# Queries and keys of the first units in smaller transfers, and a new order of small steps in the attention ramp

## The chip, the cores and the metric

The kernel runs on one core of a Trainium2 chip. The metric is the device time of one execution in microseconds. The kernel before took 631.29 us, the median of 3 runs (631.18 to 631.58). The profiled execution took 631.73 us.

## The reference

All is float32. Attention over 576 positions, for 2 batches and 8 heads of width 64, sees a window of the last 64 positions. Its output, 1152 tokens by 512, goes through a two-layer network with a softplus, and then through four gated experts with a relu.

```
scores = where(0 <= i - j < 64, q @ k.T / 8, -1e9)
attn   = exp(scores - max);  attn /= sum(attn) + 1e-9
x      = attn @ v                                  # 1152 x 512
h = x @ w_in                                       # 512 -> 2048
y = (max(h, 0) + log1p(exp(-|h|))) @ w_out         # 2048 -> 512
p = probs / (sum(probs) + 1e-9)
out = sum over e of p[:, e] * (max(y @ w1[e], 0) @ w2[e])   # 512 -> 1024 -> 512, 4 experts
```

## The kernel before, in words

**Precision.** A matrix product of the two networks is made of three: each operand is split into a high part (rounded to the format fp32r) and a low part (the rest), and high x high, high x low and low x high are summed. So each operand costs a copy (the high part) and a subtraction (the low part) before TensorE can use it: `split_up` and `up_high` make them for the first layer's weights (`wa`), `split_down` for the second's (`wb`), `x_high` and `x_low` for the attention's output, `hidden_high` and `hidden_low` for the hidden slices.

**Attention.** The work is cut into 24 units, each 192 query positions of one batch and two heads, in three windows of 64 (`w` = 0, 1, 2). Two units are a group of inputs: a row of it holds the queries and keys of the first unit, those of the second, and then the values of both (per partition 2560, 2560 and 3072 bytes; for 128 partitions 320, 320 and 384 KB). A unit goes through the engines so: TensorE `scores` (three products, each two passes) into a PSUM bank; VectorE `masked_scores` adds the mask and reduces to the negated maxima, window by window; ScalarE `softmax_exp`, three exponentials with row sums; GpSimd `add_eps` adds epsilon to the sums (units 2 to 8; VectorE does it for others); VectorE `row_inverse` and, up to unit 10, `normalise_first`; TensorE `transpose_probs`; ScalarE `copy_pT` out of PSUM; TensorE `weigh_values`; ScalarE `x_high`, VectorE `x_low`.

**Order.** Each engine has its own queue, written out by hand, and runs it strictly in order; semaphores join them. TensorE's list (L1137 to L1178) is: scores of units 0 to 2, transposes of 0, and then scores of unit j + 1, weighing of j - 2, transposes of j - 1, and so on. From unit 8 on, pieces of the first layer's matmuls (`start_up`) stand between. Then 48 steps follow, each a hidden slice of the first layer (`up`, 12 matmuls), the scores, transposes and weighing of a later unit while there are any, and the second layer's product of the slice three steps back (`down_width`). The experts follow, 8 times `product` (L1097) and `down_tokens` (L1121).

**Transfers.** SP issues all of them from one queue (L348 to L386). In it stand: unit 0's queries and keys, unit 1's, group 1's queries and keys, group 0's values, group 2 whole, group 1's values, group 3, the first block of `w_in` (two slices of `wa`), group 4, the second block, the first of `w_out`, and group 5, which waits for the weighing of unit 1. The third block of `w_in` takes the buffer of the first, and so waits for both low parts of its two slices.

**The other hands of the ramp.** VectorE copies the high parts of weight slices 0 to 4 behind the normalisation of units 4, 5, 7, 8 and 9 (`FIRST_SPLIT`), and GpSimd makes their low parts in halves (`up_low_half`, L433, called from L452 to L465); in the same loop stands `add_eps(unit + 1)`, behind the half. ScalarE and VectorE split slices 5, 6 and 7 in steps 1, 3 and 4 (`LATE_SPLIT`). In the first three steps (`LAG`) ScalarE makes the previous hidden slice's high part between the exponential and the logarithm of its own step, and VectorE its low part ahead of `relu_ln`.

Of the kernel before, what the change touches and what calls it, by code (L numbers as in the profile page):

```python
# [10 lines left out]
P = 128  # L11
# [10 lines left out]
FT = FB // P  # L22
# [9 lines left out]
N_WARM = 8  # L32
SLOTS = 3
EARLY = 2
SPLIT_GROUPS = 2
Q_COLS = 2 * 3 * P
K_COLS = 2 * (UNIT + WIN)
UNIT_QK = 3 * P + UNIT + WIN
SLOT = Q_COLS + K_COLS + 6 * P
LAG = 3  # L40
# [14 lines left out]
def two_stage_mlp_after_window_attention(nc, units, w_in, w_out, probs, w1, w2, out):  # L55
    ctx = ExitStack()
    with ctx:
# [3 lines left out]
        def sem(name):  # L61
            return ctx.enter_context(nc.semaphore(name))
# [147 lines left out]
        def score_bank(u):  # L210
            return ps_score[u % 2 if u < ALT_SCORED else 0]

        def pT_bank(u):
            return ps[3] if u < ALT_UNITS and u % 2 else ps_pT

# [24 lines left out]
        raw_a_in = [sem(f"raw_a_in{j}") for j in range(2)]  # L240
        raw_b_in = [sem(f"raw_b_in{j}") for j in range(2)]
        unit_landed = [sem(f"unit_landed{i}") for i in range(SLOTS + EARLY)]
        scores_landed = [sem(f"scores_landed{g}") for g in range(SPLIT_GROUPS)]
        first_unit_landed = sem("first_unit_landed")
        gate_in = sem("gate_in")
        out_sent = sem("out_sent")
        warm_zero = sem("warm_zero")
        consts = sem("consts")
        score_done = sem("score_done")
        negmax_done = sem("negmax_done")  # L250
        first_maxima = sem("first_maxima")
        exp_done = sem("exp_done")
        eps_done = sem("eps_done")
# [39 lines left out]

        FIRST_SPLIT = {4: 0, 5: 1, 7: 2, 8: 3, 9: 4}
        EPS_AHEAD = range(2, SCORED - 1)
        LATE_SPLIT = {1: 5, 3: 6, 4: 7}

        def f32(ap):
            return ap.bitcast(F32)
# [11 lines left out]
        def _(sp):  # L311

            def attention_inputs(g):
                s = slot_of(g)
                if g >= SLOTS + EARLY:
                    sp.wait_ge(pv_done, 2 * before_in_slot(g) + 2)
                sp.dma_start(slots[s], units[g]).then_inc(unit_landed[s], 16)

            QK = Q_COLS + K_COLS

            def first_queries_keys(g):
                sp.dma_start(slots[g][:, 0:QK], units[g][:, 0:QK]).then_inc(scores_landed[g], 16)

            def first_values(g):
                sp.dma_start(slots[g][:, QK:SLOT], units[g][:, QK:SLOT]).then_inc(unit_landed[g], 16)
# [19 lines left out]
            def down_in(b):  # L345
                return lambda j: w_out[4 * b + j]

            sp.dma_start(slots[0][:, 0:UNIT_QK], units[0][:, 0:UNIT_QK]).then_inc(first_unit_landed, 16)  # L348
            sp.dma_start(slots[0][:, UNIT_QK:2 * UNIT_QK], units[0][:, UNIT_QK:2 * UNIT_QK]).then_inc(scores_landed[0], 16)
            first_queries_keys(1)  # L350
            first_values(0)
            attention_inputs(2)
            first_values(1)
            attention_inputs(3)
            up_weights(0, up_in(0), (0,))
            attention_inputs(4)
# [41 lines left out]
        def _(pool):  # L398
# [51 lines left out]
            for u in (2, 3, 4):  # L450
                add_eps(u)
            for i, unit in enumerate((4, 5, 6, 7)):  # L452
                if unit in FIRST_SPLIT:
                    pool.wait_ge(wa_hi, FIRST_SPLIT[unit] + 1)
                else:
                    pool.wait_ge(norm_done, unit + 1)
                up_low_half(i // 2, i % 2)
                add_eps(unit + 1)
            for i, unit in zip(range(len(FIRST_SPLIT) - 1, 2 * len(FIRST_SPLIT) - 2), (8, 9, 9, 9)):
                pool.wait_ge(norm_done, unit + 1)  # L460
                if i == 4:
# [17 lines left out]
        def _(act):  # L479
# [116 lines left out]
            for k in range(STEPS):  # L596
                n, f = k // FT, k % FT
                if k < LAG:
                    copy_pT(k + WEIGHED)
                absolute(n, f)  # L600
                if LAG <= k < N_UNITS - WEIGHED:
                    copy_pT(k + WEIGHED)
                exponential(n, f)
                if k > 0:
                    hidden_high((k - 1) // FT, (k - 1) % FT)
                logarithm(n, f)
                if k < LAG:
                    x_high(k + WEIGHED)
                if k < N_UNITS - SCORED:
                    softmax_exp(k + SCORED)  # L610
                if LAG <= k < N_UNITS - WEIGHED:
                    x_high(k + WEIGHED)
                if k in LATE_SPLIT:
                    act.wait_ge(wa_hi, LATE_SPLIT[k])
                    split_up(0, LATE_SPLIT[k])
                if 0 < k - LAG + 1 < FT:
                    split_down(0, k - LAG + 1)
                if n == NCH - 1:
                    split_up(1, f)
                if 0 <= k - (NCH - 1) * FT - LAG - 1 < FT:  # L620
                    split_down(1, k - (NCH - 1) * FT - LAG - 1)
                if k in B_STEPS:
                    b_high(B_STEPS[k])
                if n == NB1 * NCH - 1:
                    a_high(f // 4, f % 4)
# [36 lines left out]
        def _(dve):  # L662
# [9 lines left out]

            def masked_scores(u):

                dve.wait_ge(score_done, u + 1)
                if u >= 3:
                    dve.wait_ge(pT_done, u - 2)
                c, half, _ = unit_place(u)
                first = (2 * c + half) % 3 == 0
                for w in range(3):  # L680
                    m = 0 if first and w == 0 else 1
                    e = dve.tensor_tensor_reduce(prob[:, u % 3, w, :], score_bank(u)[:, P * w:P * w + P],
                                                 mask[:, m, :], -SCALE, BIG, ALU.add, ALU.min,
                                                 negmax[:, u % 3, w:w + 1])
                    if u == 0 and w < 2:
                        e.then_inc(first_maxima, 1)
                e.then_inc(negmax_done, 1)
# [201 lines left out]
            for k in range(STEPS):  # L889
# [2 lines left out]
                    masked_scores(k + SCORED)  # L892
                if k < LAG:
                    rounded(n, f)
                    if k > 0:
                        hidden_low((k - 1) // FT, (k - 1) % FT)
                    relu_ln(n, f)
                    x_low(k + WEIGHED)
                    row_inverse(k + SCORED)
                    if k == 0:  # L900
                        normalise_first(SCORED)
                else:
                    rounded(n, f)
                    hidden_low((k - 1) // FT, (k - 1) % FT)
                    relu_ln(n, f)
                    if k + SCORED < N_UNITS:
                        row_inverse(k + SCORED)
                    if k + WEIGHED < N_UNITS:
                        x_low(k + WEIGHED)
# [85 lines left out]
        def _(pe):  # L995
            def scores(u):
                s = slot_of(u // 2)
                if u == 0:
                    pe.wait_ge(first_unit_landed, 16)
                elif u < 2 * SPLIT_GROUPS:  # L1000
                    pe.wait_ge(scores_landed[u // 2], 16)
                else:
                    pe.wait_ge(unit_landed[s], arrived(u // 2))
                if u >= 2:
                    pe.wait_ge(negmax_done, last_of_score_bank(u))
                for w in range(3):
                    m = pe.matmul(score_bank(u)[:, P * w:P * w + P], q_slots[s][:, u % 2, w, :],  # L1007
                                  k_slots[s][:, u % 2, WIN * w:WIN * w + P], start=True, stop=True)
                m.then_inc(score_done, 1)

            def transpose_probs(u):
# [223 lines left out]
```

## Time and profile before

| | |
|---|---|
| median of 3 runs | 631.29 us |
| profiled execution | 631.73 us |
| its span, first to last instruction | 629.9 us |
| TensorE busy | 622.1 us (99%) |
| VectorE busy | 387.6 us (62%) |
| ScalarE busy | 276.5 us (44%) |
| GpSimd busy | 89.4 us (14%) |

The span is the time from the first to the last instruction of the profiled execution; 1.8 us lie around it. Busy shares are means over all stages. Times of the rows further down count from the start of the span. The granted clock of TensorE is 1.000 over the whole span.

### The profile page before, as it was taken

The numbers are of one execution on the slowest core, as the hardware profiler recorded it, in microseconds if no ns is written. First come the engines' busy times: TensorE is split into PE (matmuls) and PEld (weight loads), VectorE is DVE, ScalarE is ACT, GpSimd is POOL, SyncE is SP. The second block draws the span as 40 slices with busy tenths as digits, with TensorE's granted clock in tenths as the row PEclk, the third lists the DMA queues.
The fourth block names the chain that finished last, engine by engine and source line by source line (L and its number), as shares of the span: only waits on it lengthen the run. The fifth ranks groups of instructions, "written<-read, shape, count | busy, mean of one in ns | idle before, by whom it ended". The sixth has DMA issues, their size and how long they took to land.

```text
span 629.9 us, 10144 instructions
## 1 busy us (share of the span) xinstructions
PE 622.1 (99%) x3892; PEld 579.5 (92%) x3892; DVE 387.6 (62%) x840; ACT 276.5 (44%) x635; POOL 89.4 (14%) x92
## 2 busy tenths in 40 slices
PE   8999999999999999999999999999999999999998
PEld 7889999999999999998998988988988988988987
DVE  5897674577646588887277277276276376376342
ACT  6886765566445455552342332332332432432410
POOL 2563333323333332000000000000000000000000
PEclk9999999999999999999999999999999999999999
DMA  8824230124100011022002103003003003000012
GB/s 325 328 93 194 68 135 1 35 100 137 65 2 0 1 35 34 1 68 101 35 0 101 34 1 103 32 1 110 25 1 119 15 2 130 5 0 1 1 51 100
DMA packets 10704, 40.78 MB, mean 65 GB/s; under 512 B 1312, under 2 KB 1568, under 8 KB 9376
## 3 DMA queue, kind: packets, MB, share of 16 engines
q1 hardware_dynamic: 10656, 40.13, 17.7%
q8 instruction: 31, 0.51, 0.3%
q14 instruction: 17, 0.14, 0.1%
HBM read 37.77 MB, written 2.36 MB: 64 GB/s over the span
## 4 chain that ended last, share of the span: by engine, by line
PE 96%; DMA 1%; ACT 1%; DVE 1%; issue 0%; POOL 0%; SPq 0%; DVEq 0%
PE banks L1121 31%; PE banks L1097 28%; PE banks L1046 16%; PE banks L1066 16%; PE banks L1007 2%; DMA unit_in<-in_units 1%; PE banks L1033 1%; PE banks L1020 1%; PE banks L1113 0%; ACT prob L498 0%; DVE prob L703 0%; POOL wa_lo L435 0%; ACT probT L507 0%; DVE wa_hi L868 0%; DVE rinv L698 0%
## 5 line engine op out<-in xcount | busy, mean ns | idle before, releaser
L1121 PE MATMUL banks<-wb_hi,ehid_hi 128*128 128x512 f32 x284 | 110.5, 389 | 0.0
L1121 PE MATMUL banks<-wb_lo,ehid_hi 128*128 128x512 f32 x284 | 110.5, 389 | 0.0
L1121 PE MATMUL banks<-wb_hi,ehid_lo 128*128 128x512 f32 x284 | 110.5, 389 | 0.0
L431 POOL TENSOR_TENSOR sp_c<-sp_e,sp_c 128x384 f32<-128x384 f32 x48 | 64.2, 1337 | 133.7 <-DVE sp_c L718 133.7
L860 DVE SCALAR_TENSOR_TENSOR part<-banks,gate,part 128x512 f32<-128x512 f32 x62 | 46.6, 751 | 54.0 <-PE banks L1121 54.0
L1097 PE MATMUL banks<-T_lo,aop_hi 128*128 128x288 f32 x256 | 75.6, 295 | 0.0
L1097 PE MATMUL banks<-T_hi,aop_lo 128*128 128x288 f32 x256 | 75.6, 295 | 0.0
L1097 PE MATMUL banks<-T_hi,aop_hi 128*128 128x288 f32 x256 | 75.3, 294 | 0.0
L1046 PE MATMUL banks<-xy_hi,wa_hi 128*128 128x384 f32 x192 | 66.3, 345 | 0.0
L1066 PE MATMUL banks<-hid_hi,wb_hi 128*128 128x384 f32 x192 | 65.8, 342 | 0.0
L1066 PE MATMUL banks<-hid_hi,wb_lo 128*128 128x384 f32 x192 | 64.3, 335 | 0.0
L1066 PE MATMUL banks<-hid_lo,wb_hi 128*128 128x384 f32 x192 | 64.3, 335 | 0.0
L1046 PE MATMUL banks<-xy_hi,wa_lo 128*128 128x384 f32 x192 | 64.2, 335 | 0.0
L1046 PE MATMUL banks<-xy_lo,wa_hi 128*128 128x384 f32 x192 | 64.2, 334 | 0.0
L1121 PEld LDWEIGHTS banks<-wb_hi,ehid_lo 128*128 128x128 f32 x284 | 53.3, 188 | 11.1
L1121 PEld LDWEIGHTS banks<-wb_hi,ehid_hi 128*128 128x128 f32 x284 | 53.3, 188 | 10.8
L1121 PEld LDWEIGHTS banks<-wb_lo,ehid_hi 128*128 128x128 f32 x284 | 53.3, 188 | 10.7
L522 ACT ACTIVATE sp_e<-banks 128x384 f32<-128x384 f32 x48 | 23.5, 490 | 76.2 <-PE banks L1046 76.2
L1097 PE MATMUL banks<-B_hi,aop_lo 128*128 128x288 f32 x192 | 56.7, 295 | 0.0
L1097 PE MATMUL banks<-B_lo,aop_hi 128*128 128x288 f32 x192 | 56.6, 295 | 0.0
L1097 PE MATMUL banks<-B_hi,aop_hi 128*128 128x288 f32 x192 | 56.5, 294 | 0.0
L570 ACT ACTIVATE kept<-banks 128x576 f32<-128x576 f32 x16 | 10.4, 651 | 90.9 <-PE banks L1097 90.9
(106 smaller groups left out, 1248.4 us busy)
## 6 DMA issues: line engine op xcount, KB each, us to landing
unit_in<-in_units SPq DMA_DIRECT2D x8, 1024.0 KB, 5.9
raw_a<-in_w SPq DMA_DIRECT2D x16, 512.0 KB, 3.3
raw_b<-in_w SPq DMA_DIRECT2D x16, 512.0 KB, 3.3
raw_a<-in_w_in SPq DMA_DIRECT2D x8, 512.0 KB, 6.1
raw_b<-in_w_out SPq DMA_DIRECT2D x8, 512.0 KB, 4.4
part<-in_units SPq DMA_DIRECT2D x2, 1024.0 KB, 12.6
out_dram<-part SPq DMA_DIRECT2D x8, 256.0 KB, 2.1
unit_in<-in_units SPq DMA_DIRECT2D x2, 384.0 KB, 8.2
```

Source lines behind the costliest of these rows:

```text
L431: pool.tensor_tensor(sp_c[:, s, :], sp_e[:, s, :], sp_c[:, s, :], ALU.subtract).then_inc(lost_done, 1)
L522: act.activation(sp_e[:, s, :], up_bank(i - 1)[:, 0:CH], ACT.Abs).then_inc(abs_done, 1)
L570: act.activation(kept[i][:, :, :], Z[i], ACT.Copy).then_inc(p1_copied, 1)
L860: dve.scalar_tensor_tensor(out=acc[:, T, :], in0=TOKEN_BANKS[T], scalar=gate[:, T, e:e + 1], in1=acc[:, T, :], op0=ALU.mult, op1=ALU.add). ...
L1007: m = pe.matmul(score_bank(u)[:, P * w:P * w + P], q_slots[s][:, u % 2, w, :], k_slots[s][:, u % 2, WIN * w:WIN * w + P], start=True, stop ...
L1020: m = pe.transpose(pT_bank(u)[:, P * w:P * w + P], prob[:, u % 3, w, :], ident[:, :])
L1033: m = pe.matmul(o_bank(u)[D * h:D * h + D, WIN * w:WIN * w + WIN], v_slots[s][:, w, c:c + D], probT[:, u % 2, w, WIN * h:WIN * h + WIN], s ...
L1046: m = pe.matmul(bank[:, 0:CH], wa[a][:, f, k, :], xy[x][:, c, k, :], start=(k == 0 and i == 0), stop=(k == KT - 1 and i == 2))
L1066: m = pe.matmul(sums[t][:, 0:CH], wb[a][:, f, P * t:P * t + P], hid[x][:, f, :], start=(f == 0 and i == 0), stop=(f == FT - 1 and i == 2))
L1097: m = pe.matmul(into[:, s, :], aop[a][:, i, row, k, :], bop[name][b][:, k, HC * s:HC * s + HC], start=(fresh and k == 0 and j == 0), stop= ...
L1121: m = pe.matmul(TOKEN_BANKS[T], ehid[x][:, i, P * T:P * T + P], wb[a][:, f, :], start=(i == 0 and j == 0), stop=(i == 3 and j == 2))
```

## The change

The queries and keys of units 2 and 3 come in a transfer each, as those of units 0 and 1 do. Group 2's queries and keys come apart from its values, and stand ahead of group 1's values. The three score blocks of unit 0 go to three PSUM banks, and each has a semaphore step, so that VectorE can reduce the first while TensorE writes the next. In GpSimd's loop `add_eps(unit + 1)` stands ahead of the wait for the weight slice and of its low half. In steps 1 and 2 the previous hidden slice's high part comes behind the exponentials of the softmax, and its low part behind `row_inverse`. Slices 5, 6 and 7 are split in steps 3, 4 and 5.

```diff
-SPLIT_GROUPS = 2
+SPLIT_GROUPS = 3
+SINGLE = 4
...
+        def score_block(u, w):
+            bank = (score_bank(0), ps[1], ps[2])[w] if u == 0 else score_bank(u)
+            return bank[:, P * w:P * w + P]
...
-        LATE_SPLIT = {1: 5, 3: 6, 4: 7}
+        LATE_SPLIT = {3: 5, 4: 6, 5: 7}
...
+            def unit_queries_keys(u):
+                cols = slice(UNIT_QK * (u % 2), UNIT_QK * (u % 2) + UNIT_QK)
+                sp.dma_start(slots[u // 2][:, cols], units[u // 2][:, cols]).then_inc(unit_scores_landed[u], 16)
...
-            sp.dma_start(slots[0][:, 0:UNIT_QK], units[0][:, 0:UNIT_QK]).then_inc(first_unit_landed, 16)
-            sp.dma_start(slots[0][:, UNIT_QK:2 * UNIT_QK], units[0][:, UNIT_QK:2 * UNIT_QK]).then_inc(scores_landed[0], 16)
-            first_queries_keys(1)
+            for u in range(SINGLE):
+                unit_queries_keys(u)
             first_values(0)
-            attention_inputs(2)
+            first_queries_keys(2)
             first_values(1)
+            first_values(2)
             attention_inputs(3)
...
             for i, unit in enumerate((4, 5, 6, 7)):
+                add_eps(unit + 1)
                 if unit in FIRST_SPLIT:
                     pool.wait_ge(wa_hi, FIRST_SPLIT[unit] + 1)
                 else:
                     pool.wait_ge(norm_done, unit + 1)
                 up_low_half(i // 2, i % 2)
-                add_eps(unit + 1)
...
                 exponential(n, f)
-                if k > 0:
+                if k >= LAG:
                     hidden_high((k - 1) // FT, (k - 1) % FT)
                 logarithm(n, f)
                 if k < LAG:
                     x_high(k + WEIGHED)
                 if k < N_UNITS - SCORED:
                     softmax_exp(k + SCORED)
+                if 0 < k < LAG:
+                    hidden_high((k - 1) // FT, (k - 1) % FT)
...
-                dve.wait_ge(score_done, u + 1)
+                if u > 0:
+                    dve.wait_ge(score_done, u + 1)
...
+                    if u == 0 and w < 2:
+                        dve.wait_ge(first_scores, w + 1)
+                    elif u == 0:
+                        dve.wait_ge(score_done, 1)
+                    e = dve.tensor_tensor_reduce(prob[:, u % 3, w, :], score_block(u, w),
...
                     rounded(n, f)
-                    if k > 0:
-                        hidden_low((k - 1) // FT, (k - 1) % FT)
                     relu_ln(n, f)
                     x_low(k + WEIGHED)
                     row_inverse(k + SCORED)
+                    if k > 0:
+                        hidden_low((k - 1) // FT, (k - 1) % FT)
...
-                if u == 0:
-                    pe.wait_ge(first_unit_landed, 16)
+                if u < SINGLE:
+                    pe.wait_ge(unit_scores_landed[u], 16)
                 elif u < 2 * SPLIT_GROUPS:
-                    pe.wait_ge(scores_landed[u // 2], 16)
+                    pe.wait_ge(scores_landed, 16)
...
+                    if u == 0 and w < 2:
+                        m.then_inc(first_scores, 1)
```

## Rows read from the trace of the kernel before

**Rows 1.** Chain of waits, first 45 us; columns: start, duration in us, what.
```profile
2.57 9.02 DMA unit_in<-in_units
```
**Rows 2.** Timeline of TensorE: start, us, line, operation, tiles, passes, idle before and releaser.
```profile
4.61 2.29 PE L1007 MATMUL banks<-unit_in 128*128 128x128 f32 x12
8.14 0.94 PE L1007 MATMUL banks<-unit_in 128*128 128x128 f32 x6 [1.23 <-DMA unit_in<-in_units]
...
15.08 0.94 PE L1007 MATMUL banks<-part 128*128 128x128 f32 x6
...
18.78 0.55 PE L1020 MATMUL banks<-ident,prob 128*128 128x128 f32 x3 [0.31 <-DVE prob L703]
...
21.11 0.55 PE L1020 MATMUL banks<-ident,prob 128*128 128x128 f32 x3 [0.44 <-DVE prob L703]
...
31.99 0.55 PE L1020 MATMUL banks<-ident,prob 128*128 128x128 f32 x3 [0.28 <-DVE prob L703]
...
36.27 0.57 PE L1033 MATMUL banks<-probT,unit_in 128*64 128x64 f32 x12 [0.96 <-issue]
...
48.58 0.45 PE L1046 MATMUL banks<-xy_hi,wa_hi 128*128 128x384 f32 x1
```
**Rows 3.** Issues and landings of group 3 and of the first weight block.
```profile
L317 SPq DMA_DIRECT2D part<-in_units x1: 496/496/496, 3.7 to 3.7; - x1
...
DMA to landing us min/median/max: 11.4/11.4/11.4
...
L333 SPq DMA_DIRECT2D raw_a<-in_w_in x1: 811/811/811, 4.2 to 4.2; - x1
...
DMA to landing us min/median/max: 12.1/12.1/12.1
```
**Rows 4.** Timeline of VectorE.
```profile
6.26 0.29 DVE L682 CUSTOM_DVE_ANT_0 prob<-banks,mask 128x128 f32<-128x128 f32 x1 [5.28 <-PE banks L1007]
...
16.31 0.43 DVE L868 CAST wa_hi<-raw_a 128x512 fp32r<-128x512 f32 x1
...
17.95 0.18 DVE L698 RECIPROCAL rinv<-rowsum 128x3 f32<-128x3 f32 x1 [0.20 <-POOL rowsum L448]
...
20.29 0.18 DVE L698 RECIPROCAL rinv<-rowsum 128x3 f32<-128x3 f32 x1 [0.33 <-POOL rowsum L448]
...
27.58 0.66 DVE L868 CAST wa_hi<-raw_a 128x512 fp32r<-128x512 f32 x1 [0.43 <-DMA raw_a<-in_w_in]
...
31.86 1.08 DVE L732 TENSOR_TENSOR sp_l<-sp_l,sp_c 128x384 f32<-128x384 f32 x1
...
36.33 1.32 DVE L665 TENSOR_TENSOR wa_lo<-raw_a,wa_hi 128x512 fp32r<-128x512 f32 x1
...
44.38 0.68 DVE L665 TENSOR_TENSOR wa_lo<-raw_a,wa_hi 128x512 fp32r<-128x512 f32 x1
...
57.86 0.29 DVE L682 CUSTOM_DVE_ANT_0 prob<-banks,mask 128x128 f32<-128x128 f32 x1 [1.30 <-PE banks L1007]
```
**Rows 5.** Timeline of GpSimd.
```profile
19.14 0.73 POOL L435 TENSOR_TENSOR wa_lo<-raw_a,wa_hi 128x256 fp32r<-128x256 f32 x1 [1.29 <-DVE wa_hi L868]
19.96 0.23 POOL L448 TENSOR_SCALAR rowsum<-rowsum 128x3 f32<-128x3 f32 x1
```
**Rows 6.** Timeline of ScalarE.
```profile
17.52 0.40 ACT L498 ACTIVATE prob<-prob,negmax 128x128 f32<-128x128 f32 x1
...
32.97 0.53 ACT L539 ACTIVATE hid_hi<-sp_l 128x384 fp32r<-128x384 f32 x1 [0.99 <-DVE sp_l L732]
...
35.18 0.62 ACT L485 ACTIVATE wa_hi<-raw_a 128x512 fp32r<-128x512 f32 x1
35.70 0.47 ACT L507 ACTIVATE probT<-banks 128x384 f32<-128x384 f32 x1
```
**Rows 7.** Stretches: us; busy by engine (operations); granted clock, DMA share, GB/s.
```profile
3.00:6.50 3.50, 3.50 (x19) 3.50 (x19) 0.24 (x3) 0.00 (x0) 0.86 (x4) 1.00 0.83 268
7.00:10.00 3.00, 1.86 (x15) 1.76 (x15) 2.42 (x17) 2.45 (x13) 0.00 (x0) 1.00 1.04 437
```

More of the change, by code:

```diff
@@ L242, in two_stage_mlp_after_window_attention @@
         unit_landed = [sem(f"unit_landed{i}") for i in range(SLOTS + EARLY)]
-        scores_landed = [sem(f"scores_landed{g}") for g in range(SPLIT_GROUPS)]
-        first_unit_landed = sem("first_unit_landed")
+        scores_landed = sem("scores_landed")
+        unit_scores_landed = [sem(f"unit_scores_landed{u}") for u in range(SINGLE)]
         gate_in = sem("gate_in")
@@ L250, in two_stage_mlp_after_window_attention @@
         negmax_done = sem("negmax_done")
+        first_scores = sem("first_scores")
         first_maxima = sem("first_maxima")
@@ L319, in _ @@
             QK = Q_COLS + K_COLS
+            def unit_queries_keys(u):
+                cols = slice(UNIT_QK * (u % 2), UNIT_QK * (u % 2) + UNIT_QK)
+                sp.dma_start(slots[u // 2][:, cols], units[u // 2][:, cols]).then_inc(unit_scores_landed[u], 16)
             def first_queries_keys(g):
-                sp.dma_start(slots[g][:, 0:QK], units[g][:, 0:QK]).then_inc(scores_landed[g], 16)
+                sp.dma_start(slots[g][:, 0:QK], units[g][:, 0:QK]).then_inc(scores_landed, 16)
             def first_values(g):
@@ L681, in masked_scores @@
                     m = 0 if first and w == 0 else 1
-                    e = dve.tensor_tensor_reduce(prob[:, u % 3, w, :], score_bank(u)[:, P * w:P * w + P],
+                    if u == 0 and w < 2:
[3 more added lines that the diff above has]
+                    e = dve.tensor_tensor_reduce(prob[:, u % 3, w, :], score_block(u, w),
                                                  mask[:, m, :], -SCALE, BIG, ALU.add, ALU.min,
@@ L1006, in scores @@
                 for w in range(3):
-                    m = pe.matmul(score_bank(u)[:, P * w:P * w + P], q_slots[s][:, u % 2, w, :],
+                    m = pe.matmul(score_block(u, w), q_slots[s][:, u % 2, w, :],
                                   k_slots[s][:, u % 2, WIN * w:WIN * w + P], start=True, stop=True)
+                    if u == 0 and w < 2:
+                        m.then_inc(first_scores, 1)
                 m.then_inc(score_done, 1)
```

## The prediction

> **What bounds the kernel now.** I read the page, then the chain of waits, then the timelines of the first 60 us engine by engine. TensorE has work for 622 of 629.9 us. From the matmul at 36.27 on no wait of it is left in the trace, so a change to the attention ramp can move the end only by moving that moment. The chain in that stretch passes through group 2's transfer of 9.02 us, from 2.57 to 11.59 [rows 1], and near its end TensorE sits for 0.96 us before weighing unit 10 [rows 2]. Nothing else of the ramp counts unless it arrives there.
>
> Three things pin the ramp. (1) Transfers: the scores of unit 6 start at 15.08 [rows 2], and group 3, which they read, was issued at 3.66 and took 11.4 [rows 3], landing at 15.06. The first weight block landed at 4.20 + 12.1 = 16.3 [rows 3], and VectorE's first copy of it starts at 16.31 [rows 4]. Both are data held by the queue of transfers, and whatever is early before them waits for them. (2) Between 18 and 22 us TensorE waits twice for VectorE's normalised probabilities, 0.31 before unit 5's transposes (18.78) and 0.44 before unit 6's (21.11) [rows 2]. VectorE itself waits 0.20 and 0.33 for the row sums with epsilon that GpSimd adds [rows 4], and GpSimd adds them behind a 0.73 half of a weight slice (19.14, then 19.96) [rows 5]. (3) At 31 to 36 us ScalarE waits 0.99 for the first hidden slice (32.97), and behind it stand a logarithm, unit 11's exponentials, a 0.62 weight copy (35.18) and only then the copy of unit 10's transposed probabilities (35.70), for which TensorE waits [rows 6].
>
> **The change part by part.**
> *First scores in three banks.* VectorE's first reduction starts at 6.26 [rows 4]: it waits for six of the twelve passes that fill 4.61 to 6.90 [rows 2]. Released after the second it could start near 5.3, but the third block still at 6.26; the two reductions before it, 0.21 apart in step, are then done, so unit 0 is through 0.4 earlier. *Units 2 and 3 by unit.* TensorE waited 1.23 until group 1 landed (8.14) [rows 2]. Unit 2 is half of those bytes. Its landing lies between 4.6, when TensorE had unit 0, and 8.1; an estimate is 6.6. *Group 2's queries ahead of its values.* 384 KB less stand ahead of unit 4's scores, 0.9 us at the 437 GB/s of 7 to 10 us [rows 7]: 10.7 in place of 11.59 [rows 1]. By these three TensorE is 0.7 early at unit 3's transposes, and then stands before unit 6's scores: the bytes ahead of group 3 are the same 4.2 MB. ScalarE can be early by as much, but VectorE stands before the first weight copy, with unit 6's reductions queued behind it, until 16.3. I put the gain of all three at the end at nothing. The bounds are 0, since nothing behind 16.3 is released by them alone, and 0.1, should an engine start on a landing faster when it already stands before it.
>
> *What the splits do to the landings.* Two transfers more are issued, each some 0.5 of SP's time (0.496 for group 3's) [rows 3]. From 3 to 6.5 us, while SP is issuing, the queue moved 268 GB/s; from 7 us, with the issues out, 437 [rows 7]. If the issuing is the cause, 1.0 us more of it costs 1.0 x (1 - 268/437) = 0.4 us on every later landing; if it is only the start of a cold queue, nothing; and the smaller packets of one unit's rows could as well go better than the pair's, for 0.2 earlier. Range -0.2 to +0.5; I take 0.15 later, nearer to nothing, because the slow stretch shows before the backlog of issues builds.
> The Trainium skill speaks against these splits: "DMA: Bandwidth & Descriptors", section "Measured (HBM→SBUF, 128 partitions, SWDGE, issued from GpSimd)", wants a megabyte or more in one transfer for three quarters of the peak. By it four small pieces in place of two larger ones cost pace before group 3. The trace does not bear it out here: pieces of 320 to 1024 KB issued 0.5 us apart moved at 437 GB/s from 7 us on, so their fixed parts overlap; what it would cost as a mechanism of this kernel is the third rival below.
>
> *Row sums ahead of the weight halves (GpSimd).* This acts from 16.3 on. VectorE: first weight copy, unit 6's reductions and unit 2's low half as before, to 17.68; then the reciprocal at once in place of 17.95 (0.20 of idle gone, and 0.07 of start) [rows 4]; normalise, second weight copy, unit 7's reductions, unit 3's low half, all 0.27 early, ending at 19.65. Unit 6's exponentials run from 17.52 for 1.16, as before [rows 6]; GpSimd now adds epsilon at 18.85 instead of 19.96, so the reciprocal of unit 6 runs at 19.65, not 20.29 [rows 4, 5]. Unit 6's transposes follow its normalisation by the same lag: 21.11 - 0.66 = 20.45. From there TensorE has no idle that GpSimd ends; its order of matmuls carries this 0.66 to 0.68 through units 7, 8 and 9. Gains of VectorE beyond it (reciprocals of units 7 and 8 would be over 1.0 early) find no taker.
> The same order holds a price: the half slice that frees the raw buffer now waits for unit 8's exponentials. It would end at 23.7 rather than 24.2, the third weight block lands 3.3 after its issue, at 27.1, and VectorE's copy of it (27.58, 0.43 idle) [rows 4] comes 0.45 early. So unit 10's reductions are early by 0.45 only, yet ScalarE reaches them at 28.73 in any case and unit 10's transposes move from 31.99 [rows 2] to 31.32.
>
> *Hidden slices behind the exponentials, weight splits two steps later.* With 0.67 in hand VectorE adds the correction of slice 0 at 31.19 (31.86 before) [rows 4], reduces unit 11 to 32.9, and ScalarE, whose logarithm no longer stands behind the 0.99 wait, does the exponentials 32.97 to 34.13, the hidden slice to 34.54 (0.41 of pitch), and with the 0.62 weight copy gone the transposed copy at 34.54 to 35.01. Before it ran at 35.70 and TensorE started 0.57 later [rows 2, 6]: now 35.11. TensorE would be free at 35.31 - 0.68 = 34.63, so 0.48 of the 0.96 wait stays. The move is 36.27 - 35.11 = 1.16.
> Later uses: hidden slice 0's low part is ready near 35.7 and read at 38.7. The weight slices: the copy that was slice 6's on VectorE at 44.38 is now slice 5's, ready by 45.1 on the old clock, and TensorE wants slice 5 at 48.58 [rows 2, 4]. The last one falls into step 5, where VectorE idled 1.30 before 57.86 [rows 4] and needs 0.68. I price these at nothing; without that idle they would cost at most 0.68 once, and a gain is excluded since TensorE waits for none of them. The 1.32 taken from VectorE at 36.33 [rows 4] lets unit 12's reductions start 1.5 early, which keeps the following steps from falling behind.
>
> **Sum.** Saved 0.67 + 0.49 = 1.16, lost 0.15 by later landings: 1.0 us. The profiled execution took 631.73 with a span of 629.9, so it becomes 630.7; the median of the runs is 0.44 below it: 631.29 - 1.0 = 630.3.
>
> **Rivals.**
> 1. *Issues keep the queue slow.* All pinned starts slip by 0.4 to 0.6 instead of 0.15. For: the step from 268 to 437 GB/s once the issues are out [rows 7]. Against: it may be the mere start. Saved 0.65: 630.6.
> 2. *GpSimd's order takes the reducing engine's time.* The third weight block is held by the row sum of unit 8. If ScalarE is not ahead there, the block lands 0.2 later than before, unit 10 follows VectorE, and only the ScalarE part at 31 to 36 us is left, 0.5: 630.8. For: VectorE does stand before that block. Against: unit 8's exponentials gain 0.6 by the working above.
> 3. *The small pieces pace the queue (slower).* Each added transfer pushes all behind it by its whole issue, 2 x 0.5 [rows 3], and the slow pace lasts so much longer, 0.4 [rows 7]. Group 3 and the first weight block come 1.4 later; from 1.16 on the ramp as a whole is later than before: 631.5, slower but inside the 0.2%. The rule of the Trainium skill named above would lead here. Against: group 3 was issued at 3.66 and landed at 15.06, so 8 us and more of backlog stand between an issue and its bytes.
> 4. *Landings come earlier* by 0.2 to 0.3 as the first pieces are spread better, and the lags of VectorE are shorter than copied here: saved 1.5, 629.8.
>
> **How the numbers follow.** Forecast 0.62, rivals 0.13, 0.09, 0.05 and 0.11. A measurement of this kernel tells about 0.2% from no change, here 1.26 us: faster means below 630.03. The forecast's own range, 629.8 to 630.8, has a third of its weight below that, with rival 4 a total of 0.33. Slower by as much needs landings 2.4 later, 0.03. The rest, 0.64, is within. Range 629.5 to 631.2: it takes in rivals 1, 2 and 4, and stops short of 3.
>
> **What would show it.** Right: unit 6's scores still at 15.1 to 15.4 though unit 3's transposes end near 14.3; the first weight copy at 16.3 to 16.6 with VectorE idle before it; unit 6's transposes near 20.6; GpSimd's row sums no longer ending a VectorE wait; unit 10's weighing near 35.3 after some 0.5 of idle; unbroken TensorE after. Wrong: unit 6's scores well before 15 or after 15.6; a new wait of TensorE on a weight slice in steps 3 to 6; the 0.96 wait unshortened.

## The result, and the profile after

| | changed | before, same chips |
|---|---|---|
| median (lowest to highest) of 22 runs each, us | 632.40 (631.62 to 634.53) | 631.33 (631.07 to 632.74) |
| ratio, 95% interval | 1.0015 [1.0010, 1.0021] | |
| profiled execution, us; its span | 631.77; 630.0 | 631.73; 629.9 |

The kernel became some 1 us slower. The forecast was 630.3 with a range of 629.5 to 631.2; the measured median lies above it. Executions of one kernel often fall into groups 0.7 to 1.0 us apart and a median can jump from one group to the next, so where medians and ratio disagree (e1, e16 and e17 below) the ratio with its interval is what counts. The two profiled executions are alike, but the one of before stands 0.4 above its median and the changed one 0.6 below its own. So the pair of traces shows where time moved, and not by how much.

The page after, its head and engine totals:
```profile
span 630.0 us, 10146 instructions
...
PE 621.5 (99%) x3892; PEld 578.5 (92%) x3892; DVE 388.1 (62%) x840; ACT 277.1 (44%) x635; POOL 89.1 (14%) x92
```
TensorE after (start, duration, operation, idle before it and who ended it); it answers to [rows 2]:
```profile
7.07 0.94 PE L1024 MATMUL banks<-unit_in 128*128 128x128 f32 x6 [0.99 <-DMA unit_in<-in_units]
...
14.92 0.94 PE L1024 MATMUL banks<-part 128*128 128x128 f32 x6 [0.86 <-DMA part<-in_units]
...
18.71 0.91 PE L1024 MATMUL banks<-part 128*128 128x128 f32 x6
...
20.25 0.55 PE L1039 MATMUL banks<-ident,prob 128*128 128x128 f32 x3
...
31.72 0.55 PE L1039 MATMUL banks<-ident,prob 128*128 128x128 f32 x3 [0.86 <-DVE prob L720]
...
35.49 0.57 PE L1052 MATMUL banks<-probT,unit_in 128*64 128x64 f32 x12 [0.45 <-issue]
...
39.09 0.42 PE L1085 MATMUL banks<-hid_hi,wb_hi 128*128 128x384 f32 x1
...
41.88 0.45 PE L1065 MATMUL banks<-xy_hi,wa_hi 128*128 128x384 f32 x1
...
45.96 0.41 PE L1085 MATMUL banks<-hid_hi,wb_hi 128*128 128x384 f32 x1 [0.73 <-ACT hid_hi L549]
```
Read it from the top. Unit 2 is 1.07 earlier (7.07 for 8.14), and all but 0.16 of that is gone at unit 6's scores: 14.92 for 15.08, behind 0.86 of waiting for group 3. Unit 6's transposes are 0.86 early (20.25 for 21.11), unit 10's only 0.27 (31.72 for 31.99): a wait of 0.28 there became 0.86. Unit 10's weighing is 0.78 early, with 0.45 of idle left of 0.96. The up product at 41.88 is still 0.8 ahead of before (42.68). Then comes something new, 0.73 of idle before the second down product at 45.96.

That product is the row to watch. In before the first and the second down product start thus (TensorE):
```profile
39.90 0.42 PE L1066 MATMUL banks<-hid_hi,wb_hi 128*128 128x384 f32 x1
...
45.81 0.41 PE L1066 MATMUL banks<-hid_hi,wb_hi 128*128 128x384 f32 x1
```
In all 20 traces of this study the span less the start of this product is 584.0 to 584.1: here 629.9 - 45.81 and 630.0 - 45.96. Whatever the ramp gains or loses reaches the end through it alone. Below, D0 is the start of the first down product (39.09 here, 39.90 before) and D1 that of the second.

VectorE after, answering to [rows 4]:
```profile
16.16 0.43 DVE L885 CAST wa_hi<-raw_a 128x512 fp32r<-128x512 f32 x1 [0.93 <-DMA raw_a<-in_w_in]
...
29.85 0.74 DVE L709 TENSOR_SCALAR rowsum<-rowsum 128x3 f32<-128x3 f32 x1 [0.33 <-ACT prob L508]
...
30.84 0.83 DVE L720 TENSOR_TENSOR prob<-prob,rinv 128x384 f32<-128x384 f32 x1
...
34.84 0.18 DVE L715 RECIPROCAL rinv<-rowsum 128x3 f32<-128x3 f32 x1
35.05 0.56 DVE L754 TENSOR_TENSOR hid_lo<-sp_l,hid_hi 128x384 fp32r<-128x384 f32 x1
35.52 1.19 DVE L749 TENSOR_TENSOR sp_l<-sp_l,sp_c 128x384 f32<-128x384 f32 x1
...
39.57 1.18 DVE L749 TENSOR_TENSOR sp_l<-sp_l,sp_c 128x384 f32<-128x384 f32 x1
...
43.45 1.17 DVE L749 TENSOR_TENSOR sp_l<-sp_l,sp_c 128x384 f32<-128x384 f32 x1
...
44.53 0.68 DVE L677 TENSOR_TENSOR wa_lo<-raw_a,wa_hi 128x512 fp32r<-128x512 f32 x1
45.14 0.68 DVE L682 TENSOR_TENSOR wb_lo<-raw_b,wb_hi 128x512 fp32r<-128x512 f32 x1
```
The same engine before, where the correction (L732 there, L749 after) is quick twice:
```profile
30.70 0.17 DVE L692 TENSOR_SCALAR rowsum<-rowsum 128x3 f32<-128x3 f32 x1 [0.22 <-ACT prob L498]
...
35.77 0.18 DVE L698 RECIPROCAL rinv<-rowsum 128x3 f32<-128x3 f32 x1
35.87 0.55 DVE L732 TENSOR_TENSOR sp_l<-sp_l,sp_c 128x384 f32<-128x384 f32 x1
...
40.04 0.55 DVE L732 TENSOR_TENSOR sp_l<-sp_l,sp_c 128x384 f32<-128x384 f32 x1
...
44.99 0.68 DVE L670 TENSOR_TENSOR wb_lo<-raw_b,wb_hi 128x512 fp32r<-128x512 f32 x1
```
The second down product reads the low part of down slice 1 (wb_lo). Before, it ended at 45.67 and TensorE started 0.14 later, with no idle named: the slice arrived just in time. After, it ends at 45.82, again 0.14 ahead of TensorE. Over all 20 traces the two cases part cleanly. In eleven D1 follows the end of wb_lo by 0.14 or 0.15, and D1 - D0 is 5.91 or more; in the other nine the slice is done 0.35 to 0.41 ahead, and D1 - D0 is 5.87 to 5.90. Both traces of the kernel before are among the eleven, by a hair (5.91 and 5.94). The label "ACT hid_hi L549" on the 0.73 wait names another slice's high part, which happened to end at 45.96; five of the eight traces with a wait at this place print wb_lo instead. TensorE was free 0.8 earlier than before, VectorE was not.

GpSimd before and after, at the same times:
```profile
36.03 1.07 POOL L424 TENSOR_TENSOR prob<-prob,rinv 128x384 f32<-128x384 f32 x1 [0.32 <-DVE rinv L698]
```
```profile
29.83 1.42 POOL L452 TENSOR_TENSOR wb_lo<-raw_b,wb_hi 128x256 fp32r<-128x256 f32 x2
...
35.10 1.20 POOL L434 TENSOR_TENSOR prob<-prob,rinv 128x384 f32<-128x384 f32 x1 [0.43 <-DVE rinv L715]
39.14 1.20 POOL L434 TENSOR_TENSOR prob<-prob,rinv 128x384 f32<-128x384 f32 x1 [0.43 <-DVE rinv L715]
```
Each of these slow VectorE rows starts behind a GpSimd row that is under way: 29.85 behind 29.83, 35.52 behind 35.10, 39.57 behind 39.14. It takes 0.57 to 0.64 more than its quick form. (Before has such pairs too, elsewhere: its correction at 31.86 takes 1.08.) GpSimd starts to normalise once the reciprocal is there. Before, the correction followed the reciprocal at once (35.77, 35.87) and was under way when GpSimd came at 36.03. After, the hidden slice's low part stands between them (35.05), GpSimd starts at 35.10, and the correction at 35.52 comes second. And ScalarE, which rounds hidden slice 2, now stands for that correction:
```profile
40.78 0.53 ACT L549 ACTIVATE hid_hi<-sp_l 128x384 fp32r<-128x384 f32 x1 [0.56 <-DVE sp_l L749]
```

### The profile page after: what moved, and what is told of

Read it like the earlier page. It is cut to its first block, busy times and chain, and to the rows that moved or that the text cites. A ratio compares the mean times of both kernels' runs of the same rounds, so it can differ in the third digit from the quotient of the medians.

```text
span 630.0 us, 10146 instructions
## 1 busy us (share of the span) xinstructions
PE 621.5 (99%) x3892; PEld 578.5 (92%) x3892; DVE 388.1 (62%) x840; ACT 277.1 (44%) x635; POOL 89.1 (14%) x92
## 4 chain that ended last, share of the span: by engine, by line
PE 96%; DMA 2%; ACT 1%; SPq 1%; DVE 1%; issue 0%
PE banks L1140 31%; PE banks L1116 28%; PE banks L1065 16%; PE banks L1085 16%; DMA raw_a<-in_w_in 2%; PE banks L1052 1%; PE banks L1024 1%; PE banks L1039 1%; PE banks L1132 0%; SPq L329 0%; SPq L335 0%; ACT prob L508 0%; ACT sp_e L537 0%; DVE prob L720 0%; DVE rowsum L709 0%
```

## The experiments

Each ratio is to runs of the kernel before on the same chip. "Up slices" and "down slices" are slices of the two weight matrices.

**e1: does the moved up slice hold the down slice?** In steps 3 to 5, on ScalarE and VectorE:
```diff
+if 0 < k - LAG + 1 < FT:
+    split_down(0, k - LAG + 1)
 if k in LATE_SPLIT:
...
     split_up(0, LATE_SPLIT[k])
-if 0 < k - LAG + 1 < FT:
-    split_down(0, k - LAG + 1)
```


> The changed kernel, with the split of the down weights (split_down) ahead of the split of the late up slice in steps 3 to 5, on ScalarE and VectorE. Theory W (the new wait of TensorE before the second down product, 0.73 us at 45.96, ends with the low part of down slice 1, which VectorE makes from 45.14 to 45.82): that low part comes 0.6 earlier, the wait shrinks to 0.1 to 0.3, and the kernel is 0.5 to 0.9 faster than the changed one: some 631.6 where the changed one has 632.4. Theory H (the wait ends with a hidden high part on ScalarE, as the releaser is printed): the wait stays at 0.7 and the time too.

632.25, ratio 1.0003 [0.9994, 1.0012]. D1 - D0 is 6.25, where the changed kernel has 6.87 and before 5.91. An order of slices that brings wb_lo 0.6 forward takes 0.6 off D1 - D0 (and 0.6 off the median, by the ratios 1.3, against e2 on the same chip): the wait is for wb_lo, whatever the label says. The rest of it is still there without a label: wb_lo ends at 46.39 in e1 and D1 is 46.54. The run doesn't say why VectorE was late.

**e2: the changed kernel once more; e3: without the hidden move; e4: without the late slices.** In e3:
```diff
-if k >= LAG:
+if k > 0:
     hidden_high((k - 1) // FT, (k - 1) % FT)
 logarithm(n, f)
...
```
with the low part again ahead of relu_ln on VectorE; in e4:
```diff
-LATE_SPLIT = {3: 5, 4: 6, 5: 7}
+LATE_SPLIT = {1: 5, 3: 6, 4: 7}
```


> The changed kernel unaltered, for a second profile and for times on the same chip as the others. Its profiled execution took 631.77, near the low end of its runs (631.6 to 634.5, median 632.4), so one profile does not show all of the loss. Expected: median 632.0 to 632.8, 0.7 to 1.2 over the kernel before. Theory L (landings of the first transfers vary and pin the ramp): the extra microsecond of a slower execution shows as later landings of group 3 or of the first or third weight block. Theory W: it shows as a longer wait before the second down product, with the same landings.

> The changed kernel with the hidden slices' high and low parts of steps 1 and 2 back in their old places (ScalarE ahead of the logarithm, VectorE ahead of the relu). Theory W with its cause in this move (VectorE's corrections now run beside GpSimd's normalisation, 1.19 instead of 0.55, and push the down slice's low part back): the wait before the second down product falls below 0.3, the wait before unit 10's weighing grows back to 0.8 to 1.0, and the total is 0.2 to 0.7 faster than the changed kernel. If the move is worth what was predicted (0.4 saved at unit 10 and nothing lost later), it is 0.3 to 0.5 slower than the changed kernel.

> The changed kernel with the late up slices 5, 6 and 7 split in steps 1, 3 and 4 again. Step 3 has one up slice and one down slice on VectorE in either case, so theory W expects the wait before the second down product unchanged or longer (0.7 to 1.5) and the wait before unit 10's weighing longer by 0.5: 632.4 to 633.4. If the move of the slices is itself at fault, the time falls back to the kernel before, 631.4.

e2 632.85, 1.0023 [1.0013, 1.0033]; e3 631.90, 1.0004 [0.9996, 1.0013]; e4 632.87, 1.0019 [1.0010, 1.0027]. On one chip, undoing the hidden move alone gives 0.95 back. D1 - D0 is 6.85 in e2, 5.87 in e3 and 6.96 in e4. The wait before unit 10's weighing is 0.44 in e3 and 0.98 in e4. So the forecast's saving there belongs to the late slices, and the new wait to the hidden move.

e2's trace also shows one reason why executions of one kernel differ by 1 us. Group 4 lands at 6.4 + 13.6 = 20.0 in it; in the profile of the changed kernel it was 5.9 + 12.8 = 18.7. Issue and landing, then TensorE, in e2:
```profile
L323 SPq DMA_DIRECT2D part<-in_units x1: 437/437/437, 6.4 to 6.4; - x1
...
DMA to landing us min/median/max: 13.6/13.6/13.6
```
```profile
20.09 0.94 PE L1024 MATMUL banks<-part 128*128 128x128 f32 x6 [0.98 <-DMA part<-in_units]
```
and its queues in 16 to 17.5 us:
```profile
q8 instruction: 1, 0.02, 4.5%
```
One instruction packet takes 4.5% of 16 engines x 1.5 us, 1.08 us on one engine. That engine's share of group 4, and so its landing, comes 1.2 late. In the first profiles of both kernels it falls into 17.5 to 19 us instead, and group 4 is in time.

**e5: transfers and first scores alone; e6: before once more; e7: row sums first and late slices alone; e8: e3 with group 4's queries and keys as a transfer of their own.** e8, which e10 repeats on e7 (units 8 and 9 then wait for the first transfer alone):
```diff
-attention_inputs(4)
+sp.dma_start(slots[4][:, 0:QK], units[4][:, 0:QK]).then_inc(fourth_scores_landed, 16)
+first_values(4)
```


> The kernel before with the new transfers and the three score banks alone (row sums, hidden slices and late up slices as before). Prediction on record: nothing gained at the end, within 0.2 us of the kernel before. Theory P (in some executions a 16 KB instruction transfer of 1.05 us sits on one transfer engine and lands group 4 at 20.0 instead of 18.8; in the changed kernel unit 8's scores stand right at that landing, in the one before they have 0.37 in hand): the scores of unit 8 stand at about 19.1 here as before, so the same exposure as before and the same time, 631.3 to 631.8. If the smaller transfers cost pace by themselves, 0.3 us or more slower, with group 3 landing after 15.3.

> The kernel before unaltered: a second profile of it. The first took 631.73 where its median is 631.3 to 631.5, so part of the ramp in that profile is a slower draw. Expected: median 631.3 to 631.7; in the profile the second down product starts between 45.3 and 45.9. If an instruction transfer falls before group 4's landing here too, unit 8's scores wait 0.5 to 0.9 and the execution is near 632.5.

> The kernel before with two parts alone: the row sums ahead of the weight halves, and the up slices 5 to 7 split in steps 3 to 5. Transfers and hidden slices as before. Theory W + P: unit 6's transposes 0.6 earlier, the wait before unit 10's weighing 0.45 instead of 0.96, no wait before the second down product: 0.5 to 1.1 faster than the kernel before in executions with group 4 on time, and about even where it is late; median 630.5 to 631.3. If the extra exposure eats all of it, 631.3 to 631.8.

> The changed kernel with the hidden slices as before, and group 4's queries and keys in a transfer of their own ahead of its values. They land 0.9 ahead of the whole group, at 17.7, so even 1.2 late they are there by 18.9 and unit 8's scores (18.7) wait at most 0.3. Theory P: the spread of the runs shrinks and the median falls to 630.6 to 631.2, 0.7 or more below the same kernel without the split (631.9). If landings are not what separates the executions: 631.9 again.

e5 631.72, 1.0007 [0.9998, 1.0016]; e6 631.46, 0.9999 [0.9990, 1.0008]; e7 630.55, 0.9989 [0.9980, 0.9998]; e8 630.92, 0.9991 [0.9982, 1.0000]. Two of the four parts together are a gain: e7's interval lies below 1. The transfers bring nothing and may cost 0.4, though their interval reaches 1. Put on top of e7's two parts they read dearer: e3 is e7 with the new transfers and first scores, and its ratio is 0.0015 higher, 0.9 us, with intervals that just touch. e8 takes 0.8 of it back by the ratio. In e3 TensorE stood 0.63 for group 4 (19.33), in e8 not at all, though the whole group landed still later there.

**e9: the hidden move alone; e10: e7 with group 4 split; e11: e7 with units 2 and 3 apart; e12: e7 with group 2's queries and keys ahead.** First e11's edit, then e12's:
```diff
-first_queries_keys(1)
+sp.dma_start(slots[1][:, 0:UNIT_QK], units[1][:, 0:UNIT_QK]).then_inc(third_unit_landed, 16)
+sp.dma_start(slots[1][:, UNIT_QK:2 * UNIT_QK], units[1][:, UNIT_QK:2 * UNIT_QK]).then_inc(scores_landed[1], 16)
...
-attention_inputs(2)
+first_queries_keys(2)
 first_values(1)
+first_values(2)
```


> The kernel before with the move of the hidden slices' high and low parts alone. Theory W: VectorE's corrections of slices 1 and 2 fall beside GpSimd's normalisations (1.19 instead of 0.55 each), the down slice's low part ends some 0.6 to 1.1 later than 45.7 of the profile before, and TensorE waits for it before the second down product by as much; the wait before unit 10's weighing stays at 0.96, since the up slice of step 1 still stands on ScalarE: 0.5 to 1.1 slower than the kernel before. Prediction on record: faster by up to 0.1, no wait at the second down product.

> The best so far (row sums first, slices later, transfers and hidden slices as before; 630.55) with group 4's queries and keys in a transfer of their own. Theory P: fewer slow executions, median 630.2 to 630.6 and the highest run under 631.4. If one more transfer costs what theory S says (0.2 each of later landings), 630.5 to 630.8.

> The best so far (630.55) with the queries and keys of units 2 and 3 in a transfer each: one more issue. Theory S (each transfer added ahead of group 3 lands everything behind it 0.2 later): first weight block at 15.9 to 16.1 on average, median 630.7 to 631.0, 0.1 to 0.4 slower than the best so far. If splitting costs nothing: 630.4 to 630.7.

> The best so far (630.55) with group 2's queries and keys ahead of its values: one more issue, and group 1's values ahead of group 2's. Theory S: as for the units apart, 630.7 to 631.0. If only the number of small packets counts (units of 2560 bytes), this one is the cheaper of the two: 630.5 to 630.7.

e9 632.52, 1.0016 [1.0007, 1.0025]; e10 630.57, 0.9983 [0.9975, 0.9992]; e11 631.00, 0.9993 [0.9983, 1.0004]; e12 630.97, 0.9992 [0.9983, 1.0001]. The hidden move alone costs as much as the whole change. Its trace has both halves of the finding, the old wait before the weighing unshortened and the new one behind it:
```profile
36.42 0.57 PE L1035 MATMUL banks<-probT,unit_in 128*64 128x64 f32 x12 [0.98 <-issue]
...
46.98 0.41 PE L1068 MATMUL banks<-hid_hi,wb_hi 128*128 128x384 f32 x1 [0.83 <-ACT hid_hi L539]
```
e10 beats both kernels. In it group 4's queries and keys landed at 17.2 while its values landed at 19.6, so unit 8's scores no longer wait for the late share. e11 and e12 read some 0.3 over e7 by the ratios, not resolved from it.

**e13: the hidden move on ScalarE alone; e14: on VectorE alone; e15: row sums first alone; e16: late slices alone.** e15's edit:
```diff
 for i, unit in enumerate((4, 5, 6, 7)):
+    add_eps(unit + 1)
...
     up_low_half(i // 2, i % 2)
-    add_eps(unit + 1)
```


> The kernel before with ScalarE's part of the hidden move alone (high part behind the exponentials; VectorE's low part in its old place, where it now waits for it). Theory V (the cost is VectorE's order: the correction slides beside GpSimd's normalisation): 0.3 or less over the kernel before. Theory A (the cost is ScalarE's order: the high part comes later, and everything of VectorE behind it too): the most of the 1.0 us is here, 0.7 or more, with VectorE waiting for the high part ahead of the relu.

> The kernel before with VectorE's part of the hidden move alone (low part behind the reciprocal; ScalarE's high part in its old place). Theory V: the corrections of slices 1 and 2 run at 1.1 to 1.2 us beside GpSimd's normalisation, the wait before the second down product is 0.6 or more, and the kernel is 0.6 to 1.1 over the one before. Theory A: 0.3 or less.

> The kernel before with the row sums ahead of the weight halves alone. By the working on record TensorE gains 0.67 at unit 6's transposes and keeps it up to the second down product, where before the wait was nothing; VectorE's chain to the down slice gains as much only if its step 1 does: 0.3 to 0.7 faster.

> The kernel before with the up slices 5 to 7 in steps 3 to 5 alone. The run with the slices in their old steps had the wait before unit 10's weighing at 0.98 where the changed kernel has 0.45, so 0.5 of the wait is this part's: 0.3 to 0.6 faster. If it were the hidden move's, as the prediction had it, nothing.

e13 634.22, 1.0044 [1.0031, 1.0057]; e14 633.09, 1.0022 [1.0013, 1.0030]; e15 631.36, 1.0003 [0.9995, 1.0012]; e16 630.74, 0.9987 [0.9978, 0.9996]. ScalarE's half alone was expected at 0.3 or less and cost 2.8, clearly more than the whole move (1.0016): with the high part late and its low part in the old place, VectorE stands for it in steps 1 and 2 of e13,
```profile
36.29 0.56 DVE L739 TENSOR_TENSOR hid_lo<-sp_l,hid_hi 128x384 fp32r<-128x384 f32 x1 [1.48 <-ACT hid_hi L539]
```
and e14, with VectorE's order alone changed, has the slow corrections (1.18 at 36.47 and 40.96). It cost 1.4 where 0.6 to 1.1 was expected, not resolved from the whole move's 1.0. So theory V is borne out by e14 and fails on e13, and the whole move is no sum of its halves. e7's gain is e16's: the late slices bring it and the row sums nothing that can be resolved, though in e7's trace unit 6's transposes start at 19.85, at least as early as forecast.

**e17: e7 with the halves of down slice 0 held until unit 10 is normalised; e18: the same on e10.**
```diff
 pool.wait_ge(wb_hi, 1)
+pool.wait_ge(norm_done, SCORED + 1)
 down_low_half(0)
```


> Row sums first and late slices (630.55 where the kernel before had 631.34), and GpSimd waits for unit 10's normalisation before its halves of the first down slice. Theory G (VectorE's row sum of unit 10 is slowed by GpSimd's half beside it): the row sum takes 0.17, the normalisation 0.56, unit 10's transposes come 0.6 to 0.8 earlier, and of that 0.3 to 0.7 reaches the end (the copy ahead of unit 10's weighing may keep the rest): 0.3 to 0.7 under the same kernel without the wait, some 1.1 to 1.5 under the kernel before. If the two only coincide: the row sum stays at 0.7 and the time at 0.8 under the kernel before.

> The same with group 4's queries and keys in a transfer of their own. Theory G as there; theory P adds fewer slow executions: highest run under 631.2, median equal to the other or 0.1 to 0.3 under it.

e17 630.90, 0.9997 [0.9988, 1.0006]; e18 630.87, 0.9991 [0.9982, 1.0000]. VectorE and TensorE of e18:
```profile
29.43 0.17 DVE L695 TENSOR_SCALAR rowsum<-rowsum 128x3 f32<-128x3 f32 x1 [0.31 <-ACT prob L501]
...
35.07 1.17 DVE L735 TENSOR_TENSOR sp_l<-sp_l,sp_c 128x384 f32<-128x384 f32 x1 [0.77 <-POOL sp_c L433]
...
43.99 0.68 DVE L673 TENSOR_TENSOR wb_lo<-raw_b,wb_hi 128x512 fp32r<-128x512 f32 x1
```
```profile
44.82 0.41 PE L1071 MATMUL banks<-hid_hi,wb_hi 128*128 128x384 f32 x1 [1.02 <-DVE wb_lo L673]
```
The row sum is quick again (0.17), TensorE loses its waits before unit 10's transposes and weighing, and D0 comes at 37.69, 1.10 before e10's 38.79. Nothing of it arrives: D1 is 44.82 against 44.68. Both expectations (a gain of 0.3 to 0.7 over e7) missed. GpSimd, put off by the halves, hands over its product sp_c late, VectorE stands 0.77 for it, and wb_lo ends at 44.67.

## Why the prediction was wrong

**The step that failed** is the paragraph on later uses: "I price these at nothing; without that idle they would cost at most 0.68 once". It looked at up slices 5 to 7, which are indeed in time (the only idle of TensorE after 35.49 is that at 45.96), and not at down slice 1, which stands behind them on VectorE and had no slack in before. Its sentence that the 1.32 taken from VectorE "keeps the following steps from falling behind" counted the late slices alone and left out what the hidden move puts back (next paragraph). The cost of the hidden move is 0.95 undone (e3 against e2) and 1.0 alone (e9, 632.52 against 631.50). The "wrong" sign that the text named, a new wait on a weight slice in steps 3 to 6, came, but on a slice that it had not considered; "unbroken TensorE after" fell with it.

Why the move makes VectorE late can be read off one stretch, from the start of the correction of slice 0 to the end of wb_lo:

| from that correction to wb_lo, us | hidden slices as before | hidden move |
|---|---|---|
| up slices in steps 1, 3, 4 | 13.55 to 13.82 (before, e5, e6, e15) | 14.83 (e4, e9) |
| up slices in steps 3, 4, 5 | 13.01 to 13.02 (e3, e7, e8, e10, e11, e12, e16) | 14.23 (after, e2) |

The late slices shorten VectorE's stretch by 0.5 to 0.8, the move lengthens it by 1.21 (14.23 for 13.02). Of these 1.21 some 0.2 fall into the room that the slice had in e3 (done 0.35 ahead of D1 instead of 0.14), and 1.0 reaches TensorE: D1 - D0 is 6.87 for 5.87. The rows say where the 1.21 comes from. Put between the reciprocal and the correction, the low part lets GpSimd's normalisation in ahead of the correction, which takes 1.18 for 0.55 in two steps running and holds ScalarE's rounding by 0.56. The three corrections of steps 1 to 3 take 3.54 in after and 1.89 in e3, 1.65 more, of which VectorE makes up a part by standing less. e14 shows that VectorE's half suffices for the slow corrections. No run moves the low part and keeps GpSimd away, so that the collision makes all of the 1.0 is an account of the rows and not a test.

**The wait before unit 10's weighing.** Forecast: 0.48 of it stays. Measured 0.45, with the start at 35.49 for 35.11 because the transposes were late. The size was right and the cause half wrong: e3, e7 and e16 have 0.44 with the hidden slices where they were, e4 and e9 0.98 with them moved. Only the weight copy had to leave. The forecast counted both parts in one sum and never asked what the hidden move adds. The answer is nothing: from the start of the correction of slice 0 to the copy of unit 10's transposed probabilities ScalarE needs 3.32 in e3 and 3.33 in after. What the logarithm gains by not standing behind the hidden slice, ScalarE loses again waiting for unit 11's maxima (1.44 of idle before 33.34 in after).

**Row sums first.** Forecast: 0.66 to 0.68 from unit 6 to unit 10. At unit 6 it is more (0.86). It does not reach unit 10's transposes: 31.72 for 31.32. The working let this gain stop nowhere. In the trace of after the row sum of unit 10 starts 0.02 behind GpSimd's half slice and takes 0.74 for 0.17. But this is a race, and not the price of the step: in before the sum was first by 0.09, and four of the seven traces with the row sums in their old place lose it as well (e5, e9, e14, e16: 0.66 to 0.68). In e16, VectorE and then GpSimd:
```profile
30.44 0.67 DVE L692 TENSOR_SCALAR rowsum<-rowsum 128x3 f32<-128x3 f32 x1 [0.39 <-ACT prob L498]
```
```profile
30.36 1.40 POOL L442 TENSOR_TENSOR wb_lo<-raw_b,wb_hi 128x256 fp32r<-128x256 f32 x2
```
The profile of before, on which the working stood, had the lucky draw. e15 measures the step at nothing; where the gain goes in the executions without a profile was not shown.

**Landings.** Group 3 was to land 0.15 later and landed at 14.87 for 15.06 in the profile. Over all traces the first weight block lands at 15.96 to 16.69 in the seven kernels with the changed transfers and at 15.54 to 16.29 in the others but e13 and e15, of which below. The 16.29 is the profile of before itself; the eight other traces with its transfers unchanged ahead of that block have 15.54 to 15.85. So the forecast pinned the ramp on a late draw, and on the mean the block comes 0.5 later with the changed transfers where 0.15 was forecast, as late as in rival 1. Stretches of the changed kernel, which answer to [rows 7]:
```profile
3.00:6.50 3.50, 3.08 (x21) 2.75 (x20) 1.10 (x9) 1.13 (x6) 0.87 (x4) 1.00 0.92 223
7.00:10.00 3.00, 2.85 (x30) 2.53 (x30) 2.57 (x16) 2.72 (x14) 0.00 (x0) 1.00 1.02 417
```
The kernels that split units 2 and 3 moved 211 to 247 GB/s in 3 to 6.5 us (e11 225), those that don't, e12 with group 2 split among them, 268 to 295. So the slow pace goes with the single units' pieces rather than with the count of issues, and rival 1 had the size and not the cause. The cost at the end is up to 0.4 on the kernel before (e5), not resolved from none, and 0.9 on e7 (e3). A slip that bears on nothing: the 4.2 MB that the prediction puts ahead of group 3 include group 3 itself. That the early scores bring nothing at the end was right. The slower rival, each issue pushing all behind it by its length, did not happen: no landing moved by 1.4.

**The sum.** Late slices -0.8 (e16), row sums 0 (e15), transfers up to +0.4 (e5), hidden move +1.0 (e9) make +0.6, all by the ratios; measured from the ratio, 0.0015 x 631.3 = 0.95 [0.6, 1.3]. The gap is within the intervals, but the parts also don't simply add: the transfers cost more once TensorE comes to unit 8 early and stands there for group 4. The forecast added the gains of the first 36 us and let them run to the end. They had to pass D1, and D1 is set by VectorE.

## What to carry to other kernels

Follow a gain to the last point where the ramp still waits for anything, and check there every input, also those that arrive just in time and so show no idle: a gain of one engine ends at the first input of another that has no slack. Moving work behind other work on an engine changes what it runs beside, and a duration from a row holds only while its neighbours do. One profile is one draw: a landing or a race within 0.1 us that a working stands on wants a second trace. Where an engine's wait has an odd label, compare its end with the ends of all that it reads.

## What the runs showed of the hardware

**VectorE beside GpSimd.** The correction, an operation on two SBUF tensors of 128x384, took 0.55 alone and 1.16 to 1.19 close behind the start of a GpSimd operation, a 128x3 row sum 0.17 and 0.66 to 0.74. The row sum ended at 30.59, when the first of GpSimd's two halves (1.42 for both, from 29.83) must have ended near 30.5. The corrections at 35.52, 39.57 and 43.45 ended 0.41, 0.41 and 0.42 after the normalisation that each lay behind (35.10, 39.14, and one of 0.83 from 43.37). That looks like blocking, not sharing. The Trainium skill says so ("SBUF — State Buffer", "Who interferes with whom": the one that issues first has the shared ports for its whole instruction, and the other is blocked); the trace agrees, with 0.57 to 0.64 added.

**An instruction packet delays a landing.** It takes 1.02 to 1.09 us on one engine in 18 of the traces, and the share of a transfer on that engine lands late, by 1.2 in e6, where fifteen engines were through with group 4 at 18.06 and the last at 19.22. In the twelve traces in which the packet starts at 16.6 to 17.4 us, group 4 lands at 19.2 to 20.1; in the five in which it starts at 17.6 or later and nothing else is late, at 18.2 to 18.8. What decides when the packet comes stays open, and so does how often it does in the executions without a profile.

**A late share stays late.** In e4, e13 and e15 the packet starts when fifteen shares of group 4 are in already. There one engine's share of group 1 (in e4, of unit 2's part of it) landed 0.5, 0.8 and 1.1 behind the fifteen others, and one share of groups 3 and 4 came late by the same amounts: group 4 at 19.2, 19.0 and 19.3. What held it at the start stays open.

**TensorE's clock.** In e13 and e15 that late share made TensorE stand for 2.1 us before unit 2's scores, where it stands 1.23 in before. TensorE of e15, and its granted clock (last but two) in two stretches:
```profile
8.66 1.47 PE L1007 MATMUL banks<-unit_in 128*128 128x128 f32 x6 [2.13 <-DMA unit_in<-in_units]
```
```profile
7.00:10.00 3.00, 1.34 (x7) 1.34 (x8) 1.28 (x7) 1.77 (x10) 0.00 (x0) 0.81 1.03 428
10.00:15.00 5.00, 5.00 (x49) 4.48 (x48) 3.99 (x24) 3.78 (x17) 0.32 (x2) 0.77 1.03 427
```
From 9 to 11 us it was 0.50 in both, 1.2 GHz, and from 13 us full again; in the other 18 traces it is 1.00 there. So these two traces are late early on, and their verdicts rest on the timed runs and on lengths, not on places.
